# Transposing the attention probabilities of two batches in 32x32 blocks on VectorE, moved by DMAs through DRAM, with the heads' steps on other halves

## What is computed

```python
scores = q @ k.T / sqrt(64)            # 4 batches, 12 heads, 448 x 448
attn = softmax(cap * tanh(scores / cap))
x = (attn @ v), heads side by side      # 1792 tokens x 768
h = sigmoid(x @ w_gate) * (x @ w_val)   # 768 -> 1536, twice
z = h @ w_out                           # 1536 -> 768
g = z @ w_in;  g = g * cos(g)           # 768 -> 2048
y = g @ moe2_w_out                      # 2048 -> 768
```

## Time and profile before

| what | value |
|---|---|
| median of 3 runs | 1243.42 us (1242.71 to 1244.03) |
| profiled execution: time, span | 1244.47 us, 1242.7 us |
| TensorE matmul busy | 1230.1 us (99%) |
| VectorE, ScalarE, GpSimd busy | 641.2 (52%), 518.5 (42%), 409.7 us (33%) |
| DMA, queue of SP | 97,200 packets, 272.51 MB, 64.1% of 16 engines |

### The profile page before, as it was taken

One profiled execution on the slowest core, in us unless ns is written; L12 is line 12 of the kernel. 1 busy time (PEld: TensorE's weight loads), 2 busy tenths in 40 slices (PEclk: granted clock), 3 DMA queues, 4 the chain that ended last, 5 costly groups with the idle time before them and its releaser, 6 DMA issues.

```text
span 1242.7 us, 17210 instructions
## 1 busy us (share of the span) xinstructions
PE 1230.1 (99%) x6232; PEld 1119.2 (90%) x6232; DVE 641.2 (52%) x1334; ACT 518.5 (42%) x1053; POOL 409.7 (33%) x410
## 2 busy tenths in 40 slices
PE   7999999999999999999999999999999999999999
PEld 5779999999899999999999999999999999999998
DVE  8951168866762126876665112787666411104610
ACT  8941156565541116556642113665564111104510
POOL 7969968799554002322012300334100000000000
PEclk9999999999999999999999999999999999999999
DMA  5579986799578665567645766556665466666763
GB/s 163 156 253 322 313 298 232 263 323 339 213 279 280 222 209 194 171 213 241 233 160 204 244 212 207 187 187 228 221 214 178 150 221 221 211 220 213 244 233 113
DMA packets 100884, 279.13 MB, mean 225 GB/s; under 512 B 11328, under 2 KB 20288, under 8 KB 100800
## 3 DMA queue, kind: packets, MB, share of 16 engines
q1 hardware_dynamic: 97200, 272.51, 64.1%
q10 hardware_dynamic: 3600, 5.51, 1.2%
HBM read 218.99 MB, written 58.98 MB: 224 GB/s over the span
## 4 chain that ended last, share of the span: by engine, by line
PE 94%; DVE 3%; ACT 2%; issue 1%; DMA 0%; SPq 0%; ACTq 0%
PE acc L629 26%; PE acc L628 26%; PE acc L630 26%; PE t_ps L580 3%; PE acc L618 2%; PE s_ps L543 2%; PE s_ps L544 2%; PE acc L598 2%; PE acc L620 2%; PE t_ps L564 1%; DVE rowmax L1141 0%; PE t_ps L582 0%; ACT prob L795 0%; DVE rowmax L994 0%; DMA qk_in_whole<-qk 0%
## 5 line engine op out<-in xcount | busy, mean ns | idle before, releaser
L628 PE MATMUL acc<-h_hi,w_hi 128*128 128x448 f32 x672 | 251.1, 374 | 0.0
L629 PE MATMUL acc<-h_lo,w_hi 128*128 128x448 f32 x672 | 245.7, 366 | 0.0
L630 PE MATMUL acc<-h_hi,w_lo 128*128 128x448 f32 x672 | 245.3, 365 | 0.0
L628 PE MATMUL acc<-x_hi,w_hi 128*128 128x448 f32 x576 | 211.3, 367 | 0.0
L630 PE MATMUL acc<-x_hi,w_lo 128*128 128x448 f32 x576 | 210.7, 366 | 0.0
L629 PE MATMUL acc<-x_lo,w_hi 128*128 128x448 f32 x576 | 210.7, 366 | 0.0
L1078 DVE SCALAR_TENSOR_TENSOR acc<-scratch,acc 128x448 f32<-128x448 f32 x48 | 30.2, 628 | 232.1 <-PE acc L630 232.0
L628 PE MATMUL acc<-z_hi,w_hi 128*128 128x448 f32 x384 | 140.2, 365 | 0.0
L630 PE MATMUL acc<-z_hi,w_lo 128*128 128x448 f32 x384 | 140.2, 365 | 0.0
L629 PE MATMUL acc<-z_lo,w_hi 128*128 128x448 f32 x384 | 140.2, 365 | 0.0
L630 PEld LDWEIGHTS acc<-h_hi,w_lo 128*128 128x128 f32 x672 | 126.3, 188 | 10.0
(11 more groups left out here) (111 smaller groups left out, 2022.3 us busy)
## 6 DMA issues: line engine op xcount, KB each, us to landing
w_lo<-w_pair SPq DMA_DIRECT2D x156, 384.0 KB, 3.8
w_hi<-w_pair SPq DMA_DIRECT2D x156, 384.0 KB, 3.1
w_lo_whole<-w SPq DMA_DIRECT2D x52, 384.0 KB, 3.9
w_pair<-w_lo SPq DMA_DIRECT2D x52, 384.0 KB, 4.5
w_pair<-w_hi SPq DMA_DIRECT2D x52, 384.0 KB, 5.0
w_lo<-w_pair SPq DMA_DIRECT2D x36, 512.0 KB, 4.3
w_hi<-w_pair SPq DMA_DIRECT2D x36, 512.0 KB, 3.3
qk_in_whole<-qk SPq DMA_DIRECT2D x23, 512.0 KB, 5.4
```

The costliest lines, as they stand in the source:

```text
L628: e.matmul(out[:, 0:S], w_hi[u % HI][:, wb, :], a_hi[:, kb, :], start=first, stop=False)
L629: e.matmul(out[:, 0:S], w_hi[u % HI][:, wb, :], a_lo[:, kb, :], start=False, stop=False)
L630: return e.matmul(out[:, 0:S], w_lo[u % LO][:, wb, :], a_hi[:, kb, :], start=False, stop=last)
```

## The change

Batches 1 and 2 (b > 0 in the code; they carry the heads of batches 2 and 3) get another way for the probabilities. VectorE transposes a normalised group in blocks of 32 x 32 within its tile (`turn_blocks`), SP writes the result to a DRAM tensor `moved` (`write_blocks`), and six DMAs a head bring the blocks back to where the transposed matrix wants them (`read_blocks`): four of 32 partitions with 14 rows of 384 bytes each, two with rows of 128 bytes. ScalarE copies them as the high part (`moved_high`) and GpSimd makes the low part (`moved_low`), and the same 14 matmuls with V read both (`times_v_moved`), into `t_ps` instead of `acc`. The keys stand in another order in the rows, which the host matches in V (`chunks_by_quarter`). On TensorE the transposes of these batches are gone, and so are `pt_high` and `pt_low`.

The steps run from -5 to 23, with scores five groups ahead. They lie on every second half of product 1 from the seventh on, on eight of the twelve halves of product 2 (0, 2, 3, 5, 6, 8, 9, 11), and on the twelve halves of product 4. `load_pair` is cut in two, and the DMAs of the step under way (four halves back) stand in SP's queue between the low and the high part. `prob` becomes a ring of three groups. Batch 0's products, with the heads of batch 1 beside them, keep the old way, and batch 3 is untouched.

```diff
+MOVED = 2 * PAIRS
+QB = 32
+BLOCKS = S // QB
+FIRST_KEYS = (0, 3, 6, 10)
+LAST_KEYS = {2: 9, 3: 13}
+MOVED_AHEAD = NG + 1
+READS = 4 + len(LAST_KEYS)
+
+STEP_HALVES = {1: range(6, 24, 2), 2: (0, 2, 3, 5, 6, 8, 9, 11), 4: range(12)}
...
+
+    pb_hi, pb_lo, pb_whole = by_block(pt_hi, CH + 1), by_block(pt_lo, CH), by_block(pt_lo_whole, CH)
+    last_whole = [tile.rearrange("p (b j) -> p b j", j=QB) for tile in (scratch[:, 6, :], prob[:, TILES - 1, :])]
+    turned_blocks = scratch[:, 2:4, :]
+    moved = nc.dram_tensor("moved", (2, TILES, P, S), F32, kind="Internal").ap()
...
+    def ahead(b):
+        return MOVED_AHEAD if b > 0 else AHEAD
+
+    def step_of(b, stage, j, h):
+
+        if b > 0:
+            n = -MOVED_AHEAD
+            for first in STEP_HALVES:
+                if first < stage:
+                    n += len(STEP_HALVES[first])
+            at = STEP_HALVES.get(stage, ())
+            return n + at.index(2 * j + h) if 2 * j + h in at else None
...
+    def prob_at(g):
+
+        ts = GROUPS[g % NG]
+        first = ts[0] if g < NG * MOVED else moved_no(g) % 3 * 2
+        return [first + n for n in range(len(ts))]
...
+            def write_blocks(g):
+
+                pr, ts = g // NG, GROUPS[g % NG]
+                if pr >= MOVED + 2:
+                    for d in range(2):
+                        e.wait_ge(s_moved[d], 16 * READS * (pr - MOVED - 1))
+                e.wait_ge(s_blocks, moved_no(g) + 1)
+                at = moved[pr % 2, ts[0]:ts[-1] + 1, :, :].rearrange("t p s -> p t s")
+                e.dma_start(at, turned_blocks[:, 0:len(ts), :]).then_inc(s_written, 16)
+
+            def read_blocks(pr, d):
+
+                e.wait_ge(s_written, 16 * (moved_no(NG * pr + (3 if d else 1)) + 1))
+                e.wait_ge(s_pv, max(2 * (pr - 1) + d + 1, 2 * MOVED))
+                whole = moved[pr % 2, :, :, :].rearrange("t (i m) s -> m (t i) s", m=QB)[:, blocks_of(d), :]
+                for r in range(4):
+                    rows, keys_in = slice(QB * r, QB * (r + 1)), slice(QB * FIRST_KEYS[r], QB * (FIRST_KEYS[r] + CH))
+                    e.dma_start(pb_whole[rows, blocks_of(d), :, :].rearrange("p b c j -> p b (c j)"),
+                                whole[:, :, keys_in]).then_inc(s_moved[d], 16)
+                for r in LAST_KEYS:
+                    rows, keys_in = slice(QB * r, QB * (r + 1)), slice(QB * LAST_KEYS[r], QB * (LAST_KEYS[r] + 1))
+                    e.dma_start(last_whole[d][rows, :, :], whole[:, :, keys_in]).then_inc(s_moved[d], 16)
+
+            def beside(b, n):
+
+                first, (i, r) = pair_of(b, 0), divmod(n, NG)
+                if 0 <= n + MOVED_AHEAD - 2 < STEPS:
+                    write_blocks(group_of(b, n + MOVED_AHEAD - 2))
+                if r == 2 and i + 1 < PAIRS:
+                    read_blocks(first + i + 1, 0)
+                if r == 0 and 0 <= i:
+                    read_blocks(first + i, 1)
+                if r == 3 and 0 <= i + 1 < PAIRS - 2:
+                    for d in range(2):
+                        load_qk(first + i + 3, d)
+                if r in (0, 2) and 0 <= i < PAIRS - 1:
+                    load_v(first + i + 1, r // 2)
...
+                        load_low(b, stage, j, h)
+                        at_b, at_n = under_way(b, n)
+                        if at_n is not None:
+                            beside(at_b, at_n)
+                        load_high(b, stage, j, h)
...
+            def moved_low(pr, d):
+
+                at = blocks_of(d)
+                e.wait_ge(s_pbhi, 2 * (pr - MOVED) + d + 1)
+                rest(pb_lo[:, at, :, :], pb_whole[:, at, :, :], pb_hi[:, at, 0:CH, :]).then_inc(s_pblow, 1)
+                e.wait_ge(s_pblow, 2 * (pr - MOVED) + d + 1)
+                rest(pb_hi[0:D, at, CH, :], last_whole[d][D:P, :, :], pb_hi[D:P, at, CH, :]).then_inc(s_pb, 1)
+                e.wait_ge(s_pb, 2 * (pr - MOVED) + d + 1)
...
+                i, r = divmod(n, NG)
+                if r in (0, 2):
+                    moved_low(first + i, r // 2)
+                if r in (1, 2) and i + 2 < PAIRS:
+                    split_qk(first + i + 2, r - 1)
+                if r == 2 and i + 1 < PAIRS:
+                    split_v(first + i + 1, 0)
+                if r == 0 and i > 0:
+                    split_v(first + i, 1)
...
+            def times_v_moved(b, i, d):
+                pr = pair_of(b, i)
+                e.wait_ge(s_pb, 2 * (pr - MOVED) + d + 1)
+                e.wait_ge(s_v[d], pr - ALONE + 1)
+                e.wait_ge(s_o, 2 * (pr - 1 - ALONE) + d + 1)
+                if pr == MOVED:
+                    e.wait_ge(s_pt, TILES * (MOVED - ALONE))
+                if i == PAIRS // 2:
+                    e.wait_ge(s_r2, b * KF2 + KF2 - 2 + d)
+                for c in range(CH + 1):
+                    vv = v_hl[d][:, c, :, :].rearrange("p a d -> p (a d)")
+                    out = output_bank(pr, d)[:, 0:S]
+                    m = e.matmul(out, vv, pb_hi[:, blocks_of(d), c, :], start=(c == 0), stop=(c == CH))
+                    if c < CH:
+                        e.matmul(out, vv, pb_lo[:, blocks_of(d), c, :], start=False, stop=False)
+                m.then_inc(s_pv, 1)
...
                 i, r = divmod(n, NG)
-                if n + AHEAD < STEPS:
-                    g = group_of(b, n + AHEAD)
+                if n + ahead(b) < STEPS:
+                    g = group_of(b, n + ahead(b))
                     e.wait_ge(s_tanh, g)
                     scores(g, s_ps)
                 blocks(0)
-                if n == 2 * U2:
+                if b == 0 and n == 2 * U2:
                     e.wait_ge(s_r2, b * KF2 + KF2 - 2)
-                if 0 <= n + 1 < STEPS:
+                if b == 0 and 0 <= n + 1 < STEPS:
                     transposes(group_of(b, n + 1))
                 blocks(1)
                 if i >= 0 and r in (1, 3):
-                    times_v(b, i, r // 2)
+                    if b == 0:
+                        times_v(b, i, r // 2)
+                    else:
+                        times_v_moved(b, i, r // 2)
                 blocks(2)
...
+                if moved_no(g) >= 3:
+                    e.wait_ge(s_blocks, moved_no(g) - 3 + 1)
+                elif g >= NG * (ALONE + 1):
+                    e.wait_ge(s_tr, min(tiles_of(g - NG)[-1] + 1, TILES * MOVED) if moved_no(g) < 0 else TILES * MOVED)
...
 
+            def moved_high(pr, d):
+
+                at = blocks_of(d)
+                e.wait_ge(s_moved[d], 16 * READS * (pr - MOVED + 1))
+                e.activation(pb_hi[:, at, 0:CH, :], pb_whole[:, at, :, :], ACT.Copy)
+                e.activation(pb_hi[D:P, at, CH, :], last_whole[d][D:P, :, :], ACT.Copy).then_inc(s_pbhi, 1)
...
+                if pr >= MOVED and pr % PAIRS == 0:
+                    e.wait_ge(s_acc, 2 * ((pr // PAIRS - 1) * UNITS + U1))
...
+                if b > 0 and 0 <= n < STEPS and n % NG in (0, 2):
+                    moved_high(pair_of(b, n // NG), n % NG // 2)
+                if 0 <= n + ahead(b) - 1 < STEPS:
+                    exp(group_of(b, n + ahead(b) - 1))
+                if n + ahead(b) < STEPS and n != 2 * U2:
+                    tanh(group_of(b, n + ahead(b)))
+                if b == 0 and 0 <= n + 1 < STEPS:
                     pt_high(group_of(b, n + 1))
...
+            def turn_blocks(g):
+
+                of = prob_at(g)
+                e.wait_ge(*normalised(tiles_of(g)[-1]))
+                if moved_no(g) > 0:
+                    e.wait_ge(s_written, 16 * moved_no(g))
+                e.transpose(turned_blocks[:, 0:len(of), :], prob[:, of[0]:of[-1] + 1, :]).then_inc(s_blocks, 1)
...
+                if n + ahead(b) < STEPS:
+                    row_max(group_of(b, n + ahead(b)))
+                if b == 0 and 0 <= n + 1 < STEPS:
                     pt_low(group_of(b, n + 1))
+                if b > 0 and 0 <= n + ahead(b) - 2 < STEPS:
+                    turn_blocks(group_of(b, n + ahead(b) - 2))
...
-                        if heads_beside(b) and j == 0:
+                        if b == 0 and j == 0:
                             e.wait_ge(s_pt, tiles_of(group_of(b, 2 * U2))[-1] - ALONE * TILES + 1)
+                        elif heads_beside(b) and j == 0:
+                            e.wait_ge(s_written, 16 * (moved_no(group_of(b, 2 * U2 + MOVED_AHEAD - 3)) + 1))
...
+    def chunks_by_quarter(heads_of):
+
+        blocks = heads_of.reshape(len(heads_of), BLOCKS, QB, D)
+        last = list(LAST_KEYS.values())
+        order = [[first + c for first in FIRST_KEYS] for c in range(CH)] + [last + last]
+        return blocks[:, order].reshape(len(heads_of), CH + 1, P, D).transpose(0, 2, 1, 3)
```

More of the change, by code:

```diff
@@ L862, in first_product @@
                     p, u = j % 2, b * UNITS + j
[L863 to L865 removed]
+                    beside = [step_of(b, 1, j, h) if heads_beside(b) else None for h in range(2)]
+                    if beside[0] is not None:
+                        attend(b, beside[0])
```

123 lines of the change are left out of this document (70 added, 53 removed).

## The result

| kernel | median of the runs | ratio to before [95% interval] | profiled execution: time, span |
|---|---|---|---|
| before | 1243.72 us (1242.71 to 1244.30, 4 runs) | 1 | 1244.47, 1242.7 us |
| changed | 1270.37 us (1268.12 to 1275.72, 4 runs) | 1.0221 [1.0188, 1.0255] | 1271.18, 1269.4 us |

The change makes the kernel 26.7 us slower; 1259 us was forecast, in a range of 1213 to 1300. The page of the changed kernel: span, busy time by engine, and the chain by engine.

The account below looks back on a forecast made before the run. TensorE, busy 99% of the span and carrying 94% of the chain, was taken as the bound. 1244.5 - 34.2 (transposes) + 50 (stalls) = 1260.3, with the median 1.1 lower: 1259 us, range 1213 to 1300.

Parts of the forecast that it names:

- What goes: TensorE in batches 1 and 2: 150 transposes a batch go, 17.1 us each batch, 34.2 us off.
- Terms of the loop: Batches 1 and 2: copy, exp, tanh, row_max, turn, write and reads form a two-step loop, 33.4 us a pair.
- The second rival: Reads from DRAM: small packets cost 45 ns each, reads 10.5 us, 1313 us in all; chance 0.13 shared with held queue.
- smallest full-rate transfer: Reads: below 512 B at twice the bytes' time, 384-byte packets take about 36 ns, near 1286 us; chance within 0.13.
- The write: Turned blocks to DRAM: 3.1 us for one tile, 3.7 for two, bounds 2.3 and 5.
- Where the stalls are: TensorE stalls a batch: 16.9 us in product 4, 7.2 in product 2, 1 from product 3; 25 in all.
- The loop's walk: Product 4, step by step: stalls of 4.9 us before step 15, 3.9 before 17, 2.5 in 19, 5.6 in 21.
- the loop through ScalarE's order: ScalarE: moved_high ahead of exp and tanh makes each turn wait for reads of two steps before; 50 us in two batches.
- The signs: Trace if right: stalls of 2 to 6 us in products 2 and 4, batch 1 some 310 us, product 1 82 to 85.
- SP's queue holds the weights: Rival, SP: 1.33 us an issue brings product 1's weights 4 us late, 1290 to 1310; chance 0.13 shared with dear packets.
- The forecast of +16: Whole kernel: 34.2 us off for transposes and 50 us on for stalls, 1244.5 to 1260.3 us.
- its direction, for which 0.57 stood: Whole kernel: slower at 0.57, against faster 0.36 and same 0.07.

Follow-up runs that it names:

- SP's order alone: Changed kernel with SP's reads and the qk and V loads behind the high weights instead of ahead; the write stays ahead: 1263.46 us, ratio 1.0163.
- the fastest kernel: Changed kernel with scores six groups ahead, earlier q/k loads and splits, reads behind high weights, write on ScalarE, products with V at their half's end: 1234.63 us.
- the kernel with the early copy: Changed kernel with ScalarE's copy of moved probabilities for step 12 ahead of product 3's last unit: 1280.51 us, ratio 1.0278.
- six ahead: Changed kernel with scores six groups ahead instead of five, and the loads and splits of q and k moved earlier: 1249.07 us, ratio 1.0038.
- the slower kernel with the late product: Changed kernel with scores six groups ahead, earlier q/k loads and splits, reads behind high weights, and products with V at their half's end: 1264.88 us.

## Why the prediction was right, and where not

- *What goes*: right. TensorE has 5932 matmuls, 300 fewer, and only batch 0's transposes of `prob`.
- *Terms of the loop*: the turn 1.11 and 0.65 us (1.1 and 0.6 predicted), `moved_high` 1.33 + 0.58 (1.95), `moved_low` 3.08 + 1.15 (4.35), six issues in 2.9 us, at 0.48 each. The last of the six reads lands 6.5 us after the first issue at the median of the 24 heads (6.1 to 8.2; 6.5 predicted), as from 622.91 to ScalarE's copy at 629.36. Inside this term two errors may cancel: the 384-byte packets took 22 ns at the median but 33 in the mean, the 128-byte ones 15 and 19, where 25 and 15 were put in as means; that makes 4.8 us for each DMA engine instead of 3.6, so 1.7 instead of 2.9 are left for queueing and landing, if packets don't overlap. The second rival (45 ns, reads of 10.5 us) falls. The Trainium skill's rule of the smallest full-rate transfer (DMA: Bandwidth & Descriptors, Specifications) gave an estimate of 36 ns and some 8.5 us. The mean of 33 ns is near it, the landing at 6.5 us is not; and 8.5 doesn't come out of the prediction's own terms (36 ns for all packets makes 8.9 us, for the 384-byte ones alone 7.6).
- *The write*: mis-sized. 3.7 us for two tiles was taken from landings of other transfers, with 5 as the upper bound; it is 6.2 at the median. No row of before had a transfer of a known place behind a burst, and the step's own issues make that burst. Without a burst ahead it takes 2.6 to 3.7, as assumed.
- *Where the stalls are*: the size was near, in part by luck. Counted from one matmul's start to the next, less the usual 0.2 us, the stalls are 22.8 and 20.9 us in the two batches against 25, and 12.6 and 12.2 in product 4 against 16.9, but the waiting parties were not those named: the scores, which were to wait for `tanh` in most places, waited 3.2 us in all. Product 2's 6.8 us (7.2 predicted) are nearly all waits for high weights, which the prediction feared for product 1 only and as a rival; product 4's are mainly products with V, from its first steps on, and not scores. The loop's walk took the first wait at the scores of step 15 (4.9 us) and missed step 13's 3.1 us, since it began with `tanh` and not with the copy that stands behind it. And moving the copies behind `exp` and `tanh` didn't help (1272.6), so the loop through ScalarE's order, the prediction's main mechanism, was not what decided. What decided was the same chain of turn, write and read: without its wait for the write 28 us go (1242.6), with a step more of distance, and the splits moved along, 21 (1249.1), and with SP's order alone 7 (1263.5).
- *The signs*: batch 1 was to take some 310 us and took 316.56. Product 1 was to take 82 to 85 us, which could not be: its 24 halves of 3.65 us are 87.6 without any heads, it took 92.38 before with four steps and takes 100.89 now with nine.
- *SP's queue holds the weights*: put at 1.33 us an issue, at 1290 us and up. The issues stay at 0.48 us; SP is held by waits, not by slow issues. The rival was real in that weights came late (14.4 us, 1.4 of it in product 1 of batch 1) and wrong in its mechanism: they were late mainly where SP's wait for the landing stood ahead of them on top of its wait for the turn. Both edits that took the landing away (1263.5 and 1242.6) left 0 and 0.8 us of waits for them, with the turn still ahead.
- *The clock*: not in the sum at all. Some 14 us, 7.6 in batch 1 and 6.5 in batch 2, of matmuls at 0.37 us apart, most of them behind stalls of 1.8 to 4.3 us.
- The sum in retrospect: -34.2, + 43.7 of stalls, + 14.1 of slow clock, + some 3 to 4 of a slightly longer distance between matmuls = 27 or so, against 26.7 measured. It closes less well than that: the two batches themselves grew by 28.2 us, and the start before them was 1.5 us shorter (386.48 against 387.98). The forecast of +16 left out the clock term, of about the size by which it was low; its direction, for which 0.57 stood, held.

## What to carry to other kernels

An in-order queue that waits for another engine's result ahead of work that the bottleneck needs must be priced by that wait, not by its issues; what it costs is only the part that the lead of that work does not cover (152 to 162 us of waits for the turn alone cost TensorE at most 0.8 us; with 60 us for landings behind them it was 14.4). Two such waits in a row must be moved together, or the second takes over what the first gave. A new trip through DRAM is best paid in distance (a group or step more ahead), and then each queue on the way, also those not in the trip, must have its work moved by the same step: the step alone cost 11 us, with GpSimd's splits moved too it gained 21. Edits didn't add up here: the same write on ScalarE was worth nothing on one base and 30 us on another. And stalls of TensorE cost more than their length: 43.7 us of them brought 14.1 us of matmuls at the lower clock, a third on top.

## What the runs showed of the hardware

- **Clock**: after a 3.1 us stall the granted clock was 0.50 to 0.55 for 6 us (the rows above), and 2.7 us were lost on top. In the fastest kernel, whose longest wait is 1.8 us, one such stretch is left, early in product 3 of batch 2: after two stalls of 1.8 and 2.1 us, 4.7 us apart, eight matmuls start 0.37 us apart. So short stalls can be followed by the lower clock as well, and a single one of 3.1 us (536.29 in the changed kernel) need not be. What decides this is not shown.
- **VectorE and GpSimd**: VectorE's normalise (448 elements) takes 0.45 us in all 47 cases in which GpSimd is idle, and 1.32 at the median, up to 1.49, in the 37 that overlap one of its instructions:

```profile
620.25 3.06 POOL L509 TENSOR_TENSOR pt_lo<-pt_lo_whole,pt_hi 128x1344 fp32r<-128x1344 f32 x1 [70.28 <-ACT pt_hi L1005]
623.38 1.16 POOL L509 TENSOR_TENSOR pt_hi<-scratch,pt_hi 64x448 fp32r<-64x448 f32 x1
...
622.23 2.57 DVE L1180 TENSOR_SCALAR prob<-prob,recip 128x448 f32<-128x448 f32 x2
```

  The first of the two runs from 622.23 to 623.56 and ends 0.25 us after GpSimd's first instruction, the second from 623.48 to 624.80 and ends 0.26 after the next. The Trainium skill (SBUF — State Buffer, Who interferes with whom) describes an exclusive lock on a shared port pair of the two engines, held for the whole instruction; both ends, just behind GpSimd's, agree with it. In the kernel with the early copy the last `tanh` of product 3 came 2.2 us later beside such an overlap.
- **DMA**: the same 448 KB write takes 2.6 to 3.7 us with at most one transfer issued in the 4.5 us before it, and 6.0 to 7.8 behind seven to nine.
- **A slightly slower TensorE in some executions**: the same 1,224 matmuls of batch 3, untouched by any edit, took 247.96 us in the changed kernel's profile, and with six ahead 252.75, at a clock column of 1.00 in both:

```profile
991.35:1244.10 252.75, 252.75 (x1224) 229.59 (x1223) 61.01 (x101) 54.30 (x99) 0.00 (x0) 1.00 0.61 207
```

  That is 2% of distance between matmuls. Of the 14 profiled executions four show it over batch 3 (the copy behind `exp` and `tanh`, six ahead with the splits, the early copy, and the slower kernel with the late product), at 4.9 us each; the other ten have 248.1 from first to last start. It would account for spreads of some 5 us between executions of one kernel, and for as much between single profiles of two. What sets it stays open.
